# Reordering three places of a fused attention and mixture-of-experts kernel: the first tile of odd units, the weight sums of group 1, the token sums at a change of pass

## The reference

```
scale = min(|a|, 0.999) / (|a| + 1e-6)
S_t = (a_t * scale_t) * S_(t-1) + k_t v_t^T     (S complex, k v^T real)
y_t = q_t . Re(S_t)
```

## Time and profile before

| what | value |
|---|---|
| runs | 2279.48, 2281.38, 2284.01 us; median 2281.38 |
| profiled execution | 2283.22 us, its span 2281.4 us |
| granted clock of PE, mean | 0.994 of full speed |
| busy share of the span | PE 98%, PEld 91%, DVE 76%, ACT 44%, POOL 21% |
| DMA | 131.34 MB, mean 58 GB/s |

### The profile page before, as it was taken

How to read it: one execution, slowest core, us unless ns; L and a number is a source line. 1 busy time by engine, 2 the same in 40 slices (tenths; PEclk the granted TensorE clock), 3 DMA queues, 4 the chain that set the end, 5 groups by cost and what they waited for, 6 DMA issues and landing times. The chain is left out here.

```text
span 2281.4 us, 38084 instructions
## 1 busy us (share of the span) xinstructions
PE 2235.4 (98%) x13741; PEld 2081.1 (91%) x13741; DVE 1728.4 (76%) x3042; ACT 1012.3 (44%) x1716; POOL 467.8 (21%) x310
## 2 busy tenths in 40 slices
PE   5899999999999999999999999999999999999999
PEld 4799999999999889999998999999998999999998
DVE  7788888888855877776778777777777777777775
ACT  6566666566555433344334433344333433334332
POOL 0000000000000423232223322233222322233222
PEclk9899999999999999999999999999999999999999
DMA  5111111111103031111110231111110211101111
GB/s 169 39 52 53 50 50 50 50 50 50 43 29 139 28 111 56 35 49 56 55 56 28 83 111 56 46 37 55 55 55 28 84 56 56 54 30 56 55 56 28
DMA packets 70726, 131.34 MB, mean 58 GB/s; under 512 B 5512, under 2 KB 36488, under 8 KB 70536
## 3 DMA queue, kind: packets, MB, share of 16 engines
q1 hardware_dynamic: 70536, 129.14, 17.4%
HBM read 114.96 MB, written 14.16 MB: 57 GB/s over the span
## 5 line engine op out<-in xcount | busy, mean ns | idle before, releaser
L606 POOL TENSOR_TENSOR h_l<-u_s,h_h 128x512 fp32r<-128x512 f32 x192 | 246.4, 1304 | 1601.5 <-ACT h_h L863 1601.5
L1777 PE MATMUL bank<-w_h,h_h 128*128 128x384 f32 x1536 | 515.7, 336 | 5.0 <-POOL h_l L606 3.8
L1779 PE MATMUL bank<-w_h,h_l 128*128 128x384 f32 x1536 | 514.8, 335 | 0.0
L1778 PE MATMUL bank<-w_l,h_h 128*128 128x384 f32 x1536 | 514.6, 335 | 0.0
L1584 PE MATMUL bank<-x_l,w_h 128*128 128x512 f32 x1056 | 414.6, 393 | 0.0
L1583 PE MATMUL bank<-x_h,w_h 128*128 128x512 f32 x1056 | 414.4, 392 | 0.0
L1585 PE MATMUL bank<-x_h,w_l 128*128 128x512 f32 x1056 | 413.5, 392 | 0.0
L1381 DVE SCALAR_TENSOR_TENSOR acc<-bank,prob,acc 128x384 f32<-128x384 f32 x352 | 214.6, 613 | 183.7 <-PE bank L1779 181.0
L1777 PEld LDWEIGHTS bank<-w_h,h_h 128*128 128x128 f32 x1536 | 289.1, 188 | 9.0 <-POOL h_l L606 5.4
L1778 PEld LDWEIGHTS bank<-w_l,h_h 128*128 128x128 f32 x1536 | 289.0, 188 | 2.0
L852 ACT ACTIVATE p_s<-bank 128x512 f32<-128x512 f32 x96 | 57.4, 598 | 523.2 <-PE bank L1585 522.9
(11 more groups left out here) (188 smaller groups left out, 3999.1 us busy)
## 6 DMA issues: line engine op xcount, KB each, us to landing
stage<-w_ SPq DMA_DIRECT2D x48, 768.0 KB, 6.6
w_raw<-w_ SPq DMA_DIRECT2D x96, 384.0 KB, 3.6
qb<-q_in_ SPq DMA_DIRECT2D x24, 192.0 KB
kb<-k_in_ SPq DMA_DIRECT2D x24, 192.0 KB
vb<-v_in_ SPq DMA_DIRECT2D x24, 192.0 KB
x_hi<-x2h_s SPq DMA_DIRECT2D x36, 128.0 KB, 1.8
x_lo<-x2l_s SPq DMA_DIRECT2D x36, 128.0 KB, 1.8
x_h<-x_hi SPq DMA_DIRECT2D x3, 1536.0 KB, 11.3
```

Source lines behind the costliest of these rows:

```text
L606: pool.tensor_tensor(tiles_of(h_l, name), group_sum(name), tiles_of(h_h, name).bitcast(F32), ALU.subtract).then_inc(hl_done, 1)
L1777: pe.matmul(dst, h_h[:, f, t_], w2h[:, fw], start=n == 0, stop=False)
L1778: pe.matmul(dst, h_h[:, f, t_], w2l[:, fw], start=False, stop=False)
L1779: mm = pe.matmul(dst, h_l[:, f, t_], w2h[:, fw], start=False, stop=n == 3)
```

## The change

Three orders are changed; no arithmetic is.

- In odd units from 3 on, PE's `tile_in(t)` comes ahead of `p_by_tokens(u)`, which is then followed directly by `r_by_tokens(u)`.
- In group 1, DVE does `w1_sums` ahead of the sum "11_0", ACT does the three parts of `w1_hi` behind `h_hi` of "21_0", and POOL does the first two parts of `w1_lo` ahead of `h_lo` of "22_1", with the third where all three stood. `sink_rows(5)` is no longer cut in two; all five operations come at k = 2.
- At a change of pass, steps 4 and 5 of `xt_sums` (half j = 0) come at k = 5 and k = 6 of the y loop; `xt_lo` (half j = 1) stays where it was.

```diff
--- before.py
+++ after.py
@@ -592,12 +592,12 @@
                     pool.tensor_tensor(w2_piece(w2l, j, i), w2_piece(w2_raw, j, i), w2_piece(w2h, j, i).bitcast(F32),
                                        ALU.subtract).then_inc(w2_low, 1)
 
-            def w1_lo(g, j):
+            def w1_lo(g, j, parts=range(3)):
                 raw_ = quad(j)
                 h, l, to = w1s[j]
-                for part, (w, r_) in enumerate(((slice(W_11, W_22), raw_[:, :, :, 0]),
-                                                (slice(W_22, S_1), raw_[:, 1:3, :, 1]),
-                                                (slice(S_1, NW), to[:, S_1:NW]))):
+                for part in parts:
+                    w, r_ = ((slice(W_11, W_22), raw_[:, :, :, 0]), (slice(W_22, S_1), raw_[:, 1:3, :, 1]),
+                             (slice(S_1, NW), to[:, S_1:NW]))[part]
                     pool.wait_ge(w1_high, g * 3 + part + 1)
                     pool.tensor_tensor(l[:, w], r_, h[:, w].bitcast(F32), ALU.subtract).then_inc(w1_low, 1)
 
@@ -608,13 +608,16 @@
 
             def group(ex, j, nxt=True):
                 g = ex * QUADS + j
+                one = isinstance(g, int) and g == 1
                 for name in LOW:
+                    if one and name == "22_1":
+                        w1_lo(g + 1, 1 - j, range(2))
                     h_lo(g, name)
                     if isinstance(g, int) and g == 0 and name == "12_0":
                         w2_lo(0, 0)
                 if nxt or j == 0:
                     if in_sink(g):
-                        w1_lo(g + 1, 1 - j)
+                        w1_lo(g + 1, 1 - j, range(2, 3) if one else range(3))
                     w2_lo(g + 1, 1 - j)
 
             def expert(ex, nxt=True):
@@ -872,7 +875,7 @@
 
             def group(ex, j, nxt=True, x2_next=False):
                 g = ex * QUADS + j
-                zero = isinstance(g, int) and g == 0
+                zero, one = (isinstance(g, int) and g == i for i in range(2))
                 keep_p1(g, 0)
                 relu(g, "22_0")
                 h_hi(g, "22_0")
@@ -883,6 +886,9 @@
                     w2_hi(0, 0, 0)
                 keep_p1(g, 1)
                 h_hi(g, "21_0")
+                if one:
+                    for part in range(3):
+                        w1_hi(ex + j, g + 1, 1 - j, part)
                 relu(g, "22_1")
                 h_hi(g, "22_1")
                 if zero:
@@ -901,8 +907,9 @@
                     w2_hi(0, 1, 1)
                     first_y(5, PB)
                 elif nxt or j == 0:
-                    for part in range(3):
-                        w1_hi(ex + j, g + 1, 1 - j, part)
+                    if not one:
+                        for part in range(3):
+                            w1_hi(ex + j, g + 1, 1 - j, part)
                     w2_hi(ex + j, g + 1, 1 - j)
                 if x2_next:
                     xt_hi(x2_next)
@@ -1388,17 +1395,15 @@
                 sk_n[0] += 1
                 dve.wait_ge(sink, sk_n[0])
 
-            def sink_rows(r, parts=(0, 1)):
+            def sink_rows(r):
                 if r == 0:
                     dve.wait_ge(exp_done, 1)
-                if 0 in parts:
-                    chained(dve.tensor_reduce(tot[:], prob[:], AX.X, ALU.add))
-                    chained(dve.tensor_scalar(tot[:], tot[:], EPS_SUM, None, ALU.add))
-                    chained(dve.reciprocal(tot[:], tot[:]))
-                if 1 in parts:
-                    chained(dve.tensor_tensor(prob[:], prob[:], tot[:].unsqueeze(2).to_broadcast([128, CH * B, E]),
-                                              ALU.mult))
-                    chained(dve.tensor_reduce(cold[:], prob[:].rearrange("p n e -> p e n"), AX.X, ALU.add))
+                chained(dve.tensor_reduce(tot[:], prob[:], AX.X, ALU.add))
+                chained(dve.tensor_scalar(tot[:], tot[:], EPS_SUM, None, ALU.add))
+                chained(dve.reciprocal(tot[:], tot[:]))
+                chained(dve.tensor_tensor(prob[:], prob[:], tot[:].unsqueeze(2).to_broadcast([128, CH * B, E]),
+                                          ALU.mult))
+                chained(dve.tensor_reduce(cold[:], prob[:].rearrange("p n e -> p e n"), AX.X, ALU.add))
 
             def sink_columns(r):
                 dve.wait_ge(sink_pe, r + 3)
@@ -1439,6 +1444,8 @@
                 next_x2(2)
                 if second:
                     sink_columns(3)
+
+                    w1_sums(ex + j, g + 1, 1 - j)
                 sums(g, 0, ("11",))
                 if first:
                     gate_out(GROUPS - 1)
@@ -1451,11 +1458,11 @@
                 sums(g, 1, ("u2",))
                 h_lo(g, "21_0")
                 sums(g, 1, ("u4",))
-                next_x2(4)
+                if j:
+                    next_x2(4)
                 if first:
                     gate_max(1)
                 sums(g, 1, ("u3", "22"))
-                next_x2(5)
                 if first:
                     gate_max(2)
                 sums(g, 1, ("12", "11", "21"))
@@ -1465,13 +1472,13 @@
                 h_lo(g, "21_1")
                 if first:
                     sink_rows(0)
-                if second:
-                    sink_rows(5, (0,))
                 for k in range(PB):
                     if second and k == 2:
-                        sink_rows(5, (1,))
-                    if k == (2 if second else 0) and (nxt or j == 0):
+                        sink_rows(5)
+                    if not second and k == 0 and (nxt or j == 0):
                         w1_sums(ex + j, g + 1, 1 - j)
+                    if j == 0 and k in (5, 6):
+                        next_x2(k - 1)
                     if first and k in (4, 6):
                         sink_columns(k // 2 - 2)
                         sink_rows(k // 2 - 1)
@@ -1664,11 +1671,16 @@
                 if u == 2:
 
                     mm_in(0)
+                merged = u % 2 and u >= 3
+                if merged:
+
+                    tile_in(t)
                 p_by_tokens(u)
                 if u == 0:
                     first_lo(LEAD, LEAD + 1)
 
-                tile_in(t if u != 2 else 1)
+                if not merged:
+                    tile_in(t if u != 2 else 1)
                 r_by_tokens(u)
                 if u == 1:
                     first_lo(LEAD + 2, LEAD + 4)
```

## The result

In 15 runs of each kernel the changed kernel took 2284.50 us in the median (2282.99 to 2287.13) and the kernel before 2279.59 (2278.39 to 2284.01). The ratio is 1.0017, with a 95% interval of 1.0009 to 1.0025: slower by about 3.9 us, between 2 and 6 (the medians alone differ by 4.9). The forecast was +4.5. The profiled execution took 2284.53 us, with a span of 2282.7 and a mean clock of 0.996.

The account below looks back on a forecast made before the run. PE was taken to bound the attention stage, busy all 620.00 us. Odd units +7.9, pass changes -2.4, clock there -1.2 and group 1 +0.2 sum to +4.5 on 2281.38, giving 2285.9 us, range 2276.5 to 2291.5.

Parts of the forecast that it names:

- Part 1: Odd units from 3 on, first tile ahead of p: PE waits for DVE before k's transposes, +7.9 us in all.
- `by_q` starts 0.60 after them: Odd units: DVE's by_q starts 0.60 us after p's transposes, in unit 21 at 611.18 instead of 609.11.
- 4.31 us remain: Unit 21: DVE's chain from by_q to the end of by_k takes 4.31 us, without the old 0.24 wait.
- 0.77 later than before: Unit 21: PE starts k's transposes at 615.55 instead of 614.78; taken as 0.80.
- just fits: Third tile of unit 21: tile_lo of the first tile ends at 622.30, PE comes at 622.37.
- 0.8 to 0.9 us: Sign in the odd units: PE waits this long for kt before L1529, ten times.
- Part 2: Changes of pass: later token sums start POOL's chain 1.2 us earlier each, -2.4 us, and a clock fall goes, -1.2.
- Part 3: Group 1: DVE's wait for weights and its lock with POOL nearly cancel a shorter wait for cold, +0.2 us.
- below 3: Sign in group 1: PE's wait at L1710, for the row step cold, shrinks from 3.06 us to under 3.
- the chain does not reach PE: Rival at k_mul in q_and_k: DVE's chain is shorter than PE's 4.12 us, total 2277.1 us; chance 0.20.
- the clock falls in attention: Rival: new waits among the transposes lower the clock three times, +3.6, total 2289.5 us; chance 0.15 with the third tile's +2.
- the pass changes gain nothing: Rival at the changes of pass: POOL waits for something else, total 2289.5 us; chance 0.05.

Follow-up runs that it names:

- only_first_tile: The kernel before with only the odd units' new order (first tile ahead of p); 2290.44 us, ratio 1.0039 to the kernel before.
- undo_first_tile: The changed kernel with PE's order of the odd units put back, token sums and group 1 as changed; 2276.28 us, ratio 0.9976 to the kernel before.
- block_behind: The changed kernel with DVE's block step of odd units moved from before k_by_r to behind tile_lo(t - 1); 2285.67 us, ratio 1.0017 to the kernel before.
- steps_spread: The changed kernel with two odd-unit block steps moved, one behind tile_lo(t - 1), the last behind tile_lo(t); 2275.24 us, ratio 0.9974 to the kernel before.
- only_group1: The kernel before with only the new order of w1 and the row step in group 1; 2280.69 us, ratio 0.9998 to the kernel before.
- only_token_sums: The kernel before with only steps 4 and 5 of the token sums moved to the y loop; 2276.02 us, ratio 0.9981 to the kernel before.
- old_group1: The kernel before with first tile ahead of p, two block steps moved, and token-sum steps 3 to 5 late, group 1 unchanged; 2275.05 us, ratio 0.9969.
- before_spread: The kernel before with only two odd-unit block steps moved, behind tile_lo(t - 1) and tile_lo(t); 2280.69 us, ratio 0.9995 to the kernel before.
- two_blocks_ahead: The changed kernel with a second block step ahead of k_by_r in odd units; 2295.43 us, ratio 1.0058 to the kernel before.

## Why the prediction was right

**Part 1, right in mechanism and nearly in size.** The step "`by_q` starts 0.60 after them" came to 0.60, "4.31 us remain" to 4.23, the 0.06 to 0.05, "0.77 later than before" to 0.75, and the third tile, which "just fits", was at 626.76 with `tile_lo` done at 626.65. Unit 23 has no wait, as its missing block step said. The +7.9 came to +8.1 in the trace, to 9.0 by the medians of only_first_tile and 9.3 by undo_first_tile, which are known to some 3 us. That +8.1 is so near is in part luck: the ten pairs of units cost 0.87 each and not the 0.80 of the forecast, +8.7, and 0.5 came back behind unit 22, of which only 0.08 were foreseen. Unit 21 shows what 0.80 left out: PE is 0.80 late at the third tile, but 0.92 late at p of unit 22 (635.24, now 640.52, less the offset of 4.36). In between, three matmuls of a tile take 0.354 us (627.19 to 630.73, ten such threes) where they took 0.341 (622.04 to 625.45); why they do is open. The sign "0.8 to 0.9 us" of wait for `kt` stands in no bracket, which shows 0.41; it is in the starts.

**What the forecast had and was not used.** It put the end of `tile_lo` 0.07 ahead of the third tile, "which just fits". So the second deadline was as tight as the first, and the forecast's own rows said so; the number did not suffer, because both bind at the same amount. But the expectation of block_behind passed over it, and with it the advice to shorten only the chain to k, which was wrong. "After this DVE has slack that is not used up" held: in steps_spread a block step stands behind `tile_lo(t)` and PE has no later wait.

**Part 2, right.** "1.2" each was 1.18 at the first pass change, and at the second 1.2 with 1.6 for the clock, where 1.2 stood. That the clock would not fall was a guess from one trace, and it held in all ten traces with these sums moved. What PE still waits for POOL is 0.36 + 0.45 and 0.20 + 0.44 us, by the forecast "about 0.7 in each". The conversion by ACT was indeed hidden.

**Part 3, right in its small sum.** The wait for the weights was to be 1.0 and was 0.99. The lock took 1.51 - 0.42 = 1.1 from one addition. The Trainium skill, SBUF — State Buffer, Who interferes with whom, says that a DVE instruction with two SBUF inputs and a GpSimd instruction that reads SBUF hold each other up for a whole instruction. The rows agree: POOL's pair ended at 780.54 + 2.73 = 783.27, the addition at 783.54. +0.2 was forecast, and about +1 by the rule alone; +0.5 stands in the trace (+0.65 in only_group1), and -0.5 (-2.3 to +1.6) by the ratio of only_group1. That L1710's wait would fall "below 3" came true with 1.73, but that POOL would be what PE waits for instead was not in the forecast.

**The rivals.** That the chain does not reach PE fell with the ten waits. That the clock falls in attention fell with a clock of 1.00 from 115 to 715 us in the changed kernel, in block_behind and in steps_spread. That the pass changes gain nothing fell with only_token_sums.

**The whole.** +4.5 was forecast; from unit 3 on the traces differ by +4.6 (8.1 - 1.2 - 2.8 + 0.5), and the runs say +3.9, between 2 and 6.

## What to carry to other kernels

The idle time of an engine ahead of its first input is no slack when that input is what moves. Before delaying an input, list every later deadline of the engine behind it, not the first alone: relieving one hands the wait to the next, and an edit that loses by itself can gain a little (here 0.08 us a pair, in the trace alone) once the fillers between the deadlines stand behind them. Work without a deadline near (here the sums for the next pass) belongs behind the last operation for which another engine waits.

## What the runs showed that was not expected

**The clock.** The old order of group 1, in which PE waits 3.06 or 3.07 us for `cold`, had a y half of 22.86 us at a clock of 1.00 in the kernel before. In only_first_tile and in old_group1 it had (busy time by stretch):

```profile
789.10:813.10 24.00, 19.75 (x103) 18.79 (x102) 18.40 (x38) 5.90 (x9) 11.79 (x7) 0.93 0.00 1
```

```profile
782.10:807.37 25.27, 21.01 (x104) 20.03 (x102) 18.43 (x38) 5.91 (x10) 11.80 (x7) 0.86 0.00 1
```

So one and the same code lost nothing, 1.1 or 2.4 us, by whether and for how long the clock fell in that execution. Falls of this size, also in the start-up, go with the spread between runs of one kernel. The traces show where they are, but the mean clock is known for every run: of the 26 runs of the kernel before beside only_first_tile, the 13 at 0.996 or 0.997 took 2278.31 to 2282.23 us and the 4 at 0.993 took 2283.80 to 2286.27. With such a spread the last versions could not be ranked.

**Shorter waits at the pass changes, and no fall there.** In the four kernels with the old token sums (before, before_spread, only_first_tile, only_group1), where PE waits 1.4 to 1.5 and 0.4 us for POOL, the clock fell at four of the eight pass changes, each time to half for 3.4 us. In the ten kernels with the sums moved, where it waits at most 0.36 and 0.45 us, it fell at none of twenty. There is one trace of each kernel, so this is a strong sign and no proof; it would explain why the token sums gave more in time than the 2.4 us of their waits. In attention, the ten stops brought no fall in the traces of the changed kernel, only_first_tile, block_behind and two_blocks_ahead.

**Recorded waits are no measure of lost time.** The changed kernel shows 0.41 for 0.75 lost at `kt`; two_blocks_ahead shows the same 0.41 at `kt` with 1.0 more lost. A bracket counts from the shown end of the last matmul, and a transpose that is followed after 0.11 us is shown as 0.27 long, so that some 0.16 of each stop are not in it; and of two waits in a row the second shows only what the first has left.

**The spacing of the tile matmuls has two values.** Behind the third tile of an odd unit, three of them take 0.354 us in the changed kernel, block_behind and two_blocks_ahead, which stop there or just before, and 0.341 in the kernel before and in steps_spread, which don't. But the first tile of the same unit has 0.352 in the kernel before too (609.52 to 610.93, four threes), so a stop is not the only thing that brings it. It is worth about 0.1 us in a pair of units, and 0.4 in the stretch behind unit 23, and its cause was not tried.
